# Local attention of a fused kernel: blocks of 26 queries and 32 keys in place of 58 and 64

## The reference

```
q_d, k_d, v_d = means over groups of 4 positions            # 144 groups
out_up   = repeat(softmax(scale * q_d @ k_d.T) @ v_d, 4)    # group attention
mask     = abs(pos[:, None] - pos[None, :]) < 4             # 7 keys for a query
out_local = softmax(where(mask, scale * q @ k.T, -1e9)) @ v # local attention
x = out_up + out_local                                      # 2304 tokens x 512
h = x @ w_in (512 x 1024);  ln = layernorm(h * softmax(h)) * g
x = ln @ w_out (1024 x 512);  h2 = x @ w_in2 (512 x 2048)
result = (h2 * cos(h2)) @ w_out2 (2048 x 512)
```

## Time and profile before

| what | value |
|---|---|
| median of 3 runs | 694.25 us (693.75 to 695.06) |
| the profiled execution's own time | 693.08 us |
| its span | 691.3 us |
| granted TensorE clock over the span | 1.00 |

### The profile page before, as it was taken

The page is one execution under the profiler, slowest core; times in us unless marked ns, Lnnn a source line. Parts: engine busy times, 40 slices in busy tenths (PEclk is TensorE's granted clock), DMA queues, the critical chain, the costliest instruction groups (busy, mean ns, idle before and its releaser), DMA issues.

```text
span 691.3 us, 12769 instructions
## 1 busy us (share of the span) xinstructions
PE 679.0 (98%) x4783; PEld 600.2 (87%) x4783; DVE 440.2 (64%) x806; ACT 407.5 (59%) x849; POOL 233.9 (34%) x315
## 2 busy tenths in 40 slices
PE   7999999999999999999999999999999999999998
PEld 4677889889889999999989989889899989898986
DVE  7888964654562324356888888965556676655553
ACT  4669865555564656466666657654445676544444
POOL 6997763553523464501222245600000430000000
PEclk9999999999999999999999999999999999999999
DMA  8962331321100000557544253443222336322202
GB/s 299 321 185 95 117 103 45 110 80 63 38 1 1 1 1 1 183 190 259 191 159 145 108 210 110 157 148 107 107 108 106 123 135 245 123 107 106 107 1 91
DMA packets 18445, 82.77 MB, mean 120 GB/s; under 512 B 1872, under 2 KB 5968, under 8 KB 15056
## 3 DMA queue, kind: packets, MB, share of 16 engines
q1 hardware_dynamic: 18384, 81.96, 33.9%
HBM read 62.56 MB, written 19.40 MB: 119 GB/s over the span
## 4 chain that ended last, share of the span: by engine, by line
PE 94%; DVE 4%; issue 1%; ACT 1%; POOL 1%; POOLq 0%; ACTq 0%
PE ps L1586 28%; PE ps L1563 25%; PE ps L1419 15%; PE ps L1450 15%; PE ps L1434 2%; PE ps L1391 2%; PE ps L1329 1%; PE ps L1377 1%; PE ps L1459 1%; PE ps L1366 1%; PE ps L1351 1%; DVE xT L1123 1%; PE ps L1322 1%; PE ps L1341 1%; DVE turn L1264 1%
## 5 line engine op out<-in xcount | busy, mean ns | idle before, releaser
L1563 PE MATMUL ps<-y_parts,w_parts 128*128 128x384 f32 x1008 | 203.2, 336 | 0.7 <-ACT part L942 0.7
L1563 PEld LDWEIGHTS ps<-y_parts,w_parts 128*128 128x128 f32 x1008 | 180.4, 188 | 15.8 <-ACT part L942 1.1
L1586 PE MATMUL ps<-wo,g_hi 128*128 128x512 f32 x576 | 179.2, 392 | 0.0
L1586 PEld LDWEIGHTS ps<-wo,g_hi 128*128 128x128 f32 x576 | 105.8, 188 | 11.8
L1586 PE MATMUL ps<-wo,g_lo 128*128 128x512 f32 x288 | 114.3, 397 | 0.0
L956 ACT ACTIVATE turn<-h,quarter 128x384 f32<-128x384 f32 x96 | 59.0, 615 | 79.6 <-DVE h L1256 79.3
L1450 PE MATMUL ps<-ln_hi,w_split 128*128 128x384 f32 x384 | 103.2, 339 | 0.0
L1270 DVE TENSOR_TENSOR turn<-h,turn 128x384 f32<-128x384 f32 x96 | 61.7, 643 | 44.0 <-ACT turn L962 44.0
L1256 DVE TENSOR_TENSOR h<-ps,part 128x384 f32<-128x384 f32 x72 | 40.1, 557 | 56.8 <-PE ps L1563 56.6
L1419 PE MATMUL ps<-w_split,x_hi 128*128 128x512 f32 x288 | 73.0, 395 | 0.1
L606 POOL TENSOR_TENSOR y_parts<-xT,y_parts 128x768 fp32r<-128x768 f32 x17 | 32.8, 1947 | 117.5 <-ACT y_parts L831 117.5
(11 more groups left out here) (110 smaller groups left out, 971.1 us busy)
## 6 DMA issues: line engine op xcount, KB each, us to landing
w_parts<-w_kept SPq DMA_DIRECT2D x16, 1792.0 KB, 7.3
w_kept<-w_parts SPq DMA_DIRECT2D x8, 1792.0 KB, 6.7
qk_in<-in_qk SPq DMA_DIRECT2D x16, 586.0 KB, 4.4
vblk<-in_v_blocks SPq DMA_DIRECT2D x16, 384.0 KB, 5.5
v<-in_v_rows SPq DMA_DIRECT2D x16, 288.0 KB
result<-o_sb SPq DMA_DIRECT2D x18, 256.0 KB, 3.8
xT<-in_w_in SPq DMA_DIRECT2D x8, 512.0 KB, 7.8
raw_wo<-in_w_out SPq DMA_DIRECT2D x8, 512.0 KB, 5.9
```

The lines of the kernel that those rows point to most:

```text
L1563: last = nc.tensor.matmul(product_ps(s, k), w[:, m, a, c, :], y_parts[:, n, b, c, :], start=(not adds and c == 0 and m == 0 and n == 0), s ...
L1586: last = nc.tensor.matmul(o_ps(tile), g[n][:, t * P:(t + 1) * P], wo[:, p, w, f, :], start=(first and m == 0), stop=(done and m == 2))
```

## The change

KEYS becomes 32, so BLK = 26, and there are 23 blocks in 6 slots of four blocks each. Block j goes to partitions 32(j mod 4) onwards. A row of scores has 2 x 6 x 32 = 384 numbers instead of 640. In results the slots lie in three groups of 32 rows (96 of the 128 rows of the transposed probabilities and of the blocks of v), and slot s writes to bank s mod 3. All six slots go through 4 transposes of 96 columns, and step x = 2 (2 transposes, one copy) is gone; the steps are renumbered 0, 1, 2. The group scores and the group output have bank 3 to themselves. The counts of the semaphore waits follow (3 copies a pair instead of 4). The band mask is made of one 128 x 128 pattern by two instructions on POOL instead of four, and copied by four on DVE instead of one. Some waits of the tile loop now name out_added in place of gout_copied. A qk_in load has 604 columns instead of 586 and a vblk load 96 partitions of 4 KB instead of 128 of 3 KB.

```
-KEYS = 64
+KEYS = 32
 BLK = KEYS - 2 * PAD
 NBLK = -(-S // BLK)
-SLOTS = NBLK // 2
+SLOTS = -(-NBLK // 4)
-PIECE = 2 * BLK
-LAST = S - 4 * PIECE
+PIECE = 4 * BLK
+LAST = S - (SLOTS - 1) * PIECE
...
-        vblk = [place(f"vblk{n}", [P, 2, 2, 3, D]) for n in range(2)]
+        vblk = [place(f"vblk{n}", [P, 4, 4, D]) for n in range(2)]
-        prT = place("prT", [P, 6, P])
+        prT = place("prT", [P, 4, P])
...
+        def gout_ps(i):
+            return ps[:, pair_banks(i) + 3, 0:G]
+
+        def result_ps(i, s, first, count):
+            at = s // 3 * PIECE + first
+            return ps[:, pair_banks(i) + s % 3, at:at + count]
...
             def copy_probsT(i, x):
-                act.wait_ge(prT_ready, 4 * i + t_order(i).index(x) + 1)
-                if x in (0, 2):
+                act.wait_ge(prT_ready, 3 * i + t_order(i).index(x) + 1)
+                if x == 0:
...
                 if x == 0:
-                    dst, src = prT[:, 0:4, :], bank.rearrange("p (m q) -> p m q", q=P)
-                elif x == 2:
-                    dst, src = prT[0:KEYS, 4:6, :], bank[0:KEYS, 0:2 * P].rearrange("p (m q) -> p m q", q=P)
+                    dst, src = prT[0:3 * KEYS], bank[0:3 * KEYS, :].rearrange("p (m q) -> p m q", q=P)
...
             def add_scales(i):
...
+                gn = PIECE // FACTOR
+                for s, count in ((0, 3), (3, 2)):
+                    at = s // 3 * PIECE
+                    fine = ps[:, pair_banks(i):pair_banks(i) + count, at:at + PIECE].rearrange("p s (g r) -> p s g r", r=FACTOR)
...
+                fine = result_ps(i, SLOTS - 1, 0, LAST).rearrange("p (g r) -> p g r", r=FACTOR)
...
             def scores(i):
...
                 for j in range(NBLK):
-                    a, s = j % 2, j // 2
+                    a, s = j % 4, j // 4
...
             def transpose_probs(i, x):
                 if x == 0:
                     pe.wait_ge(probs_ready, i + 1)
-                    need(pe, prT_copied, 4 * (before_in_banks(i) + 1))
+                    need(pe, out_added, 3 * (before_in_banks(i) + 1))
                     for m in range(4):
-                        s = 2 * (m % 2)
-                        last = nc.tensor.transpose(t_ps(i, x)[:, m * P:(m + 1) * P],
-                                                   pr[n][:, m // 2, s:s + 2, :].rearrange("p s k -> p (s k)"), ident[:])
-                elif x == 2:
-                    for h in range(2):
-                        last = nc.tensor.transpose(t_ps(i, x)[0:KEYS, h * P:(h + 1) * P],
-                                                   pr[n][:, h, SLOTS - 1, :], ident[:])
+                        three = pr[n][:, m // 2, 3 * (m % 2):3 * (m % 2) + 3, :].rearrange("p s k -> p (s k)")
+                        last = nc.tensor.transpose(t_ps(i, x)[0:3 * KEYS, m * P:(m + 1) * P], three, ident[:])
...
             def results(i):
-                pe.wait_ge(prT_copied, 4 * i + (2 if i > 1 else 4))
+                pe.wait_ge(prT_copied, 3 * i + (2 if i > 1 else 3))
...
-                for j in range(NBLK):
-                    a, s = j % 2, j // 2
+                for j in sorted(range(NBLK), key=lambda j: j % 4):
+                    a, s = j % 4, j // 4
                     count = min(BLK, S - j * BLK)
                     for h in range(2):
-                        m = 2 * h + s // 2 if s < SLOTS - 1 else 4 + h
-                        keys = slice(s % 2 * KEYS, (s % 2 + 1) * KEYS)
-                        at = s // 2 * PIECE + a * BLK
-                        last = nc.tensor.matmul(o_ps_pair(i, s % 2, at, count)[h * D:(h + 1) * D, :],
-                                                vblk[n][keys, h, a, s // 2, :],
-                                                prT[keys, m, a * KEYS:a * KEYS + count], start=True, stop=True)
+                        m, r = 2 * h + s // 3, s % 3
+                        keys = slice(r * KEYS, (r + 1) * KEYS)
+                        last = nc.tensor.matmul(result_ps(i, s, a * BLK, count)[h * D:(h + 1) * D, :],
+                                                vblk[n][keys, m, a, :], prT[keys, m, a * KEYS:a * KEYS + count],
+                                                start=True, stop=True)
```

More of the change, by code:

```diff
@@ L149, in two_scale_attention_moe @@
         ident_bf = place("ident_bf", [P, P], BF16)
-        band = place("band", [P, KEYS])
+        band = place("band", [P, P])
         band_bf = place("band_bf", [P, SLOTS, KEYS], BF16)
@@ L369, in two_scale_attention_moe @@
         o_stored = [sem(f"o_stored{n}") for n in range(6)]
-        lmax = slice(0, 10)
-        gneg, gsum, ginv = (slice(10 + 3 * n, 13 + 3 * n) for n in range(3))
+        lmax = slice(0, 2 * SLOTS)
+        gneg, gsum, ginv = (slice(2 * SLOTS + 3 * n, 2 * SLOTS + 3 * n + 3) for n in range(3))
         def pair_columns(pair, first, count):
@@ L609, in _ @@
             nc.gpsimd.memset(band[:], 0.0).then_inc(band_steps, 1)
[L610 to L618, removed]
+            for side, base in ((-1, 0), (1, 2 * PAD)):
+                pool.wait_ge(band_steps, 1 if side < 0 else 2)
+                nc.gpsimd.affine_select(out=band[:], in_=band[:], compare_op=ALU.is_ge, fill=MASKED, base=base,
+                                        pattern=[[-side, P]], channel_multiplier=side).then_inc(band_steps, 1)
             nc.gpsimd.memset(ident[:], 0.0).then_inc(ident_steps, 1)
@@ L738, in copy_group_out @@
                 need(act, out_added, 3 * i)
-                nc.scalar.activation(goT[:], o_ps_pair(i, 2, 0, G), ACT.Copy).then_inc(gout_copied, 1)
+                nc.scalar.activation(goT[:], gout_ps(i), ACT.Copy).then_inc(gout_copied, 1)
             def split_in1(c):
@@ L1174, in _ @@
             nc.vector.tensor_copy(ident_bf[:], ident[:]).then_inc(ident_steps, 1)
-            dve.wait_ge(band_steps, 5)
-            nc.vector.tensor_copy(band_bf[:], band[:].unsqueeze(1).broadcast_to([P, SLOTS, KEYS])).then_inc(band_steps, 1)
-            dve.wait_ge(band_steps, 6)
+            dve.wait_ge(band_steps, 3)
+            for a in range(4):
+                rows = slice(a * KEYS, (a + 1) * KEYS)
+                nc.vector.tensor_copy(band_bf[rows], band[rows, rows].unsqueeze(1).broadcast_to([KEYS, SLOTS, KEYS])).then_inc(band_steps, 1)
+            dve.wait_ge(band_steps, 7)
             nc.vector.memset(band_bf[0:KEYS, 0, 0:PAD], MASKED).then_inc(band_steps, 1)
             past = S + PAD - (NBLK - 1) * BLK
-            nc.vector.memset(band_bf[KEYS:P, SLOTS - 1, past:KEYS], MASKED).then_inc(band_steps, 1)
+            a = (NBLK - 1) % 4
+            nc.vector.memset(band_bf[a * KEYS:(a + 1) * KEYS, SLOTS - 1, past:KEYS], MASKED).then_inc(band_steps, 1)
             sum_k(0)
@@ L1427, in transpose_ln @@
                 if t == 0:
-                    pe.wait_ge(gout_copied, FRONT)
+                    pe.wait_ge(out_added, 3 * FRONT)
                 if t == FREE - 1 and half:
-                    pe.wait_ge(gout_copied, PAIRS)
+                    pe.wait_ge(out_added, 3 * PAIRS)
                 need(pe, ln_lo_ready, 2 * t - 1 if t >= FREE and not half else 2 * t if t >= FREE - 1 else 2 * t + half)
@@ L1616, in laid_out @@
     padded[:, :, PAD:PAD + S, :] = v.reshape(PAIRS, 2, S, D)
-    blocks = np.zeros((PAIRS, 2, KEYS, 2, 2, 3, D), v.dtype)
+    blocks = np.zeros((PAIRS, 3, KEYS, 4, 4, D), v.dtype)
     for j in range(NBLK):
-        a, s = j % 2, j // 2
-        blocks[:, s % 2, :, :, a, s // 2, :] = padded[:, :, j * BLK:j * BLK + KEYS, :].transpose(0, 2, 1, 3)
+        for h in range(2):
+            s = j // 4
+            blocks[:, s % 3, :, 2 * h + s // 3, j % 4, :] = padded[:, h, j * BLK:j * BLK + KEYS, :]
     halves = w_in2.reshape(2, 2, P, 2, JOINS, P).transpose(4, 2, 0, 3, 1, 5)
```

75 lines of the change are left out of this document (30 added, 45 removed).

## The result

The changed kernel takes 709.12 us (median of 4 runs, 708.07 to 710.83) against 694.23 us: a ratio of 1.022 (1.019 to 1.024). The forecast was 692.2 us, with a range of 687.0 to 697.0.

A forecast was written before the change was run, and what follows sets the result against it. The prediction took PE, 98% busy at the full clock, as the bound. Its terms, -1.8 us in the tile loop and -0.2 ahead, sum to -2.0 us: from the median of 694.25 to 692.2 us, range 687.0 to 697.0.

The forecast's parts named there:

- scores, stage: PE's local score matmuls, 92 pairs of weight load and matmul per pair of heads: 0.37 us plus 0.03 against 0.59, -0.19 us.
- results, stage: PE's local result matmuls, 92 pairs in six parts: 0.94 us plus 0.02 against 0.69, +0.27 us.
- band: PE's two bf16 band matmuls go from 320 to 192 columns: -0.11 us a pair of heads.
- transposes: On PE the two transposes of step x = 2 go, 0.11 us each: -0.22 us a pair of heads.
- tile loop: Sum over the turns that pass PE's savings on: -3.0, +3.0 and -1.8 us, together -1.8 us.
- ahead of the loop: Chain over several engines up to hidden(0): -0.2 us, with bounds of -0.9 and +0.5.
- gaps inside both stages: Sign in the profile after: a PE gap within the scores or results stage would be instruction supply.
- instruction supply: Slower rival: moving PE's instruction packets shows in dense turns and ahead of the loop, +5 us, 697 us; chance 0.12.
- a falling clock: Sign in the profile after: if the clock falls, the prediction calls itself wrong; no size given.
- 12 x 31 = 0.37 us: Scores on PE: the fullest of eight parts has 12 pairs, at 31 ns each for weight loads of 32 columns.
- shared path of a row group: Slower rival: four 32-column loads in a row group take 59 ns, scores +0.15 us, whole +1.7, 695.9 us; chance 0.18.
- rival on the rate of issue: Slower rival: PE takes pairs no faster than 15 ns, scores +0.79 and results +0.69 us, 710 us; chance 0.10.

## Why the prediction was wrong

By its own steps, for one pair of heads and then the sum:

| step | forecast | measured |
|---|---|---|
| scores, stage | -0.19 us | +0.18 us |
| results, stage | +0.27 us | +0.25 us |
| band | -0.11 us | -0.09 us |
| transposes | -0.22 us | -0.22 us |
| tile loop | -1.8 us | +3.9 us |
| ahead of the loop | -0.2 us | +11.5 us |

The **results**, band and transposes terms held; in the last the split was another one, 0.14 us for the two that went and 0.08 in the other four, which had been given nothing. The waits at the head of the loop were still there, the one on DVE with 0.63 us instead of 1.12, the one on ACT with 1.00 instead of 0.86, and DVE's 0.55 us came as said. Two signs that the prediction had named came as well: gaps inside both stages, which it had given to instruction supply, and a falling clock, by which it called itself wrong.

The **scores** term failed in size and sign. Its step was "12 x 31 = 0.37 us" for the fullest part. A part can go at 34 ns or less, the engine as a whole could not follow: 92 pairs at near 9 ns are 0.80. I did weigh such a limit, but took as its price the 15 ns that the old scores sustain, and dismissed it by three starts within 30 ns. Those 15 ns were the four parts' own pace (59 / 4), no limit of issue, and the three starts were a start. The true limit lay between the two numbers. It costs 10 x 0.37 = 3.7 us against the forecast. The shared path of a row group, the rival with the nearest price, is refuted by the runs with fewer score matmuls. The page TensorE: Matmul & The Clock Gate of the Trainium skill (Part 1, on 56 against 53.3 ns) says that matmuls never start closer than about 25 ns. The trace does not agree for a divided array: 9 ns a pair.

**Instruction supply** was named as a rival at 0.12 and priced at 5 us, half of a packet's moving time in each dense turn. The mechanism was right, and the price in the loop was met (2.95 us against five times 0.6). That there were five stalls is in part luck: only two of them (at 146 and 163 us) lie in the five turns that were named, where results, group scores and scores follow one another. The other three lie in turns 2 to 4, where the transposes and a transpose_ln come between as well. What failed was the step ahead of the loop: "at most 0.9 us come out of that wait" looked only at waits on other engines, and the rival's price there used the 1.2 us that a packet is moved for. What counts is the whole way: PE begins on a packet, the next one starts to move 3.5 and 4.5 us later here, with the DMA share at 1.0, is moved in 0.9 to 1.6, and can be used 1.2 to 1.7 after that. The kernel before needs 7.3 us and more for 256 records once it is running; the changed one 3.6 and 2.2 where it stalled. The two stalls are 7.0 of the 11.5 us. The other 4.5 are taken apart in part only. 1.1 us of them were lost before the first stall (the results of pair 1 begin at 22.21 instead of 21.12 us): the load of pair 1 was in at 8.9 instead of 7.9, where the prediction had looked at the first load alone, and the clock was at the lower level from 11.4 to 14.8. 3.4 us lie between there and hidden(0), with two stretches of 6.8 us at the lower clock, in which the band's two matmuls span 0.53 us instead of 0.33, and slower turns on POOL and ACT behind them. No run here held the clock up without also changing the stalls.

In the loop each stage can be summed over all turns, from start to start, after less before: scores +4.9 us (2.95 of it the stalls), results +2.9, band -1.2, transposes -1.9, group scores -0.5, group output -0.3. That is 3.9, all that was measured. The forecast had -1.9, +3.0, -1.1 and -1.8 for the first four and nothing for the last two, in which the wait on DVE became 0.5 us shorter and two waits for ACT's copies went (0.3 us). So the miss in the loop is the scores and the stalls.

The page Runtime: NRT & Kernel Launch of the Trainium skill (instruction fetch mechanics) says that instructions are streamed in blocks of 16 KiB and that the cost of crossing a block's edge is mostly hidden. The trace agrees on the block: the stalls lie whole multiples of 256 records apart. Hidden it is in the kernel before, and not in the changed one, which used up 256 records in 2.2 to 5.7 us where it stalled.

That the total comes near the 710 us of the rival on the rate of issue is luck: its 15 ns are refuted, and it put most of the loss in the loop.

## What to carry to other kernels

Count PE's instructions before cutting matmuls smaller: many small ones side by side on a divided array are held by the engine's rate over all parts and by the packets of 256 instructions, neither of which shows as a released wait. Look for "issue" gaps inside a stage and for the DMA share around them; a dense stretch on PE is the place, full DMA engines beside it make the gap longer (4.5 us ahead of the loop of the changed kernel against 0.9 in it), and some tens of instructions more ahead of it can move the loss by several us. Where precision allows, one pair instead of two for each float32 matmul is worth more than any regrouping tried here.

## What the runs showed of the hardware

- Inside a group of equal matmuls and with nothing to wait for, PE stalled only at 189 to 193 records beyond a multiple of 256, in the changed kernel and in the nine experiments that had such stalls (all but the sorted order and the bf16 reading in the kernel before), and restarted 1.2 to 1.7 us after the last instruction packet had been moved.
- A packet of instructions started to move 3.5 to 4.5 us after PE had begun on the one before with the DMA share at 1.0 (the changed kernel's two big stalls), and 0.8 to 3.5 us with a share of at most 0.12 (its stalls in the loop).
- Float32 pairs on a divided array are taken at near 9 ns each at best (46 pairs in 0.41 us, 56 in 0.50, 92 in 0.80), bf16 pairs at 7 (46 in 0.32). What sets it was not tried.
- A pair with 64 columns of float32 weights holds its part for 59 to 60 ns whether 64 or 32 columns move (the scores before and their split form); in the results it was 69 and 78 ns in the same two kernels and 59 in the changed one.
- 92 pairs in six parts take 0.94 us in one order and 1.65 us in the other; 40 pairs in four parts take 0.69 us in both.
